# Attention mask from 12 rows of hash bits, moved by DMA, in place of 64 counted one-hot rows; values ahead of hash and fold

## The reference, cut to what matters

```python
# q, k, v: [2, 8, 768, 64]; proj: [64, 6]
q_bits = (q @ proj > 0); k_bits = (k @ proj > 0)
mask = q_bucket[:, :, :, None] == k_bucket[:, :, None, :]   # bucket: the 6 bits as a number
scores = where(mask, scale * q @ k.T, -1e9)
scores = scores - max(scores, axis=-1)
attn = exp(scores); attn = attn / (sum(attn) + 1e-9)
x = attn @ v
...
# x as [1536, 512]: the best of 8 experts by x @ w_gate + bias[modality], relu(x @ w1) @ w2,
# scaled by the gate; then softplus(x @ w_in) @ w_out
```

## Time and profile before

| what | us |
|---|---|
| median of 3 runs (788.20 to 788.98) | 788.89 |
| the profiled execution's own time | 788.01 |
| its span on the core | 786.2 |
| TensorE busy | 738.3 |
| VectorE busy | 580.2 |
| ScalarE busy | 516.8 |
| GpSimd busy | 322.9 |

### The profile page before, as it was taken

The page is one execution under the profiler, slowest core; times in us unless marked ns, Lnnn a source line. Parts: engine busy times, 40 slices in busy tenths (PEclk is TensorE's granted clock), DMA queues, the critical chain, the costliest instruction groups (busy, mean ns, idle before and its releaser), DMA issues.

```text
span 786.2 us, 13234 instructions
## 1 busy us (share of the span) xinstructions
PE 738.3 (94%) x4030; PEld 621.3 (79%) x4030; DVE 580.2 (74%) x841; ACT 516.8 (66%) x938; POOL 322.9 (41%) x281
## 2 busy tenths in 40 slices
PE   5999999999999668999999999999999999999995
PEld 4888888888889556887878887878888788878884
DVE  4999898998999646714989135278888788887884
ACT  5888888888888534635888245365656666566562
POOL 8666546664662270000000000045545664557544
PEclk9999999999999969999999999999999999999999
DMA  6453101220000251503989000023323523234221
GB/s 214 180 172 114 50 30 40 82 89 30 30 10 1 90 142 40 214 0 120 333 315 355 0 0 28 0 61 101 107 83 103 157 85 107 82 105 146 95 81 53
DMA packets 36142, 79.52 MB, mean 101 GB/s; under 512 B 4112, under 2 KB 7056, under 8 KB 36112
## 3 DMA queue, kind: packets, MB, share of 16 engines
q1 hardware_dynamic: 33328, 71.71, 27.0%
q0 software_dynamic: 1920, 6.69, 2.6%
q10 hardware_dynamic: 864, 0.76, 0.3%
HBM read 72.46 MB, written 6.68 MB: 101 GB/s over the span
## 4 chain that ended last, share of the span: by engine, by line
PE 75%; DVE 9%; ACT 7%; issue 5%; POOL 1%; DMA 1%; ACTq 1%; DVEq 0%; POOLq 0%
PE psA L1373 16%; PE psA L1300 11%; PE ps L1173 6%; PE psA L1387 6%; PE psA L1389 5%; PE psA L1388 5%; PE psA L1160 5%; PE psA L1148 5%; PE ps L1182 3%; DVE w1l L968 3%; PE ps L1320 2%; PE ps L1321 2%; PE ps L1324 2%; PE psA L1309 2%; ACT w1h L626 2%
## 5 line engine op out<-in xcount | busy, mean ns | idle before, releaser
L502 POOL TENSOR_TENSOR hres<-hexp,hres 128x512 f32<-128x512 f32 x48 | 62.2, 1296 | 323.3 <-DVE hres L1049 323.2
L821 DVE TENSOR_TENSOR pTl<-psA,pTh 128x384 fp32r<-128x384 f32 x192 | 98.0, 551 | 18.7 <-ACT pTh L573 17.7
L573 ACT ACTIVATE pTh<-psA 128x384 fp32r<-128x384 f32 x192 | 83.9, 490 | 37.5 <-PE psA L1160 36.8
L1148 PE MATMUL psA<-K,Q 128*128 128x384 f32 x384 | 92.6, 364 | 2.0 <-POOLq L408 2.0
L814 DVE TENSOR_REDUCE negmax<-psA 128x1 f32<-128x768 f32 x96 | 91.1, 948 | 2.8 <-PE psA L1148 2.8
L564 ACT ACTIVATE probs<-psA,negmax 128x768 f32<-128x768 f32 x96 | 87.0, 907 | 4.9 <-DVE negmax L814 4.1
L987 DVE SCALAR_TENSOR_TENSOR hTl<-psA,hTh 128x512 fp32r<-128x512 f32 x34 | 23.5, 692 | 90.2 <-ACT hTh L661 90.2
L738 ACT ACTIVATE habs<-psA 128x512 f32<-128x512 f32 x48 | 28.7, 598 | 81.5 <-PE psA L1373 81.4
L1160 PE MATMUL psA<-ident,probs 128*128 128x128 f32 x576 | 80.1, 275 | 0.7 <-DVE pTl L821 0.6
L1003 DVE TENSOR_TENSOR wil<-rawi,wih 128x512 fp32r<-128x512 f32 x48 | 80.2, 1673 | 0.0
L1387 PE MATMUL psA<-woh,sh 128*128 128x512 f32 x192 | 75.4, 392 | 2.4 <-DVE sl L1057 2.3
(11 more groups left out here) (165 smaller groups left out, 1665.7 us busy)
## 6 DMA issues: line engine op xcount, KB each, us to landing
w2s<-in_moe_w SPq DMA_DIRECT2D x8, 2048.0 KB, 8.9
w1s<-in_moe_w SPq DMA_DIRECT2D x8, 2048.0 KB, 9.0
rawi<-in_moe_w_in SPq DMA_DIRECT2D x48, 256.0 KB, 2.7
rawo<-in_moe_w_out SPq DMA_DIRECT2D x48, 256.0 KB, 2.8
raw<-in_qk SPq DMA_DIRECT2D x16, 384.0 KB, 3.1
vs<-in_v SPq DMA_DIRECT2D x16, 192.0 KB, 2.4
x_rows<-X SPq DMA_DIRECT2D x1, 1728.0 KB, 6.0
x_rows<-X SPq DMA_DIRECT2D x1, 1512.0 KB, 5.9
```

What stands on the lines that cost most here:

```text
L573: nc.scalar.activation(pTh[u // TPGR % 2][:, g * TPH:(g + 1) * TPH, u % TPGR * P:(u % TPGR + 1) * P], psA[2][:, g, 0:HALF].rearrange("p (t ...
L821: V.tensor_tensor(pTl[u // TPGR % 2][:, g * TPH:(g + 1) * TPH, cols], psA[2][:, g, 0:HALF].rearrange("p (t n) -> p t n", t=TPH), pTh[u // ...
L1148: last = T.matmul(psA[u % 2][:, h, 0:HALF], qs[par][:, cols], ks[par][:, h * HALF:(h + 1) * HALF], start=start, stop=not start)
```

## The change

Twelve rows take the place of the 64. The projection now has 24 columns: for a query the six projections and the six negated ones, for a key the negated and then the plain ones. `take_bits` compares with a bound for each partition and multiplies by a worth for each partition: 2^100 for query rows, 1 for key rows. The products of a query's 12 rows with a key's 12 rows add up to 2^100 times the number of bits that differ. So q is scaled by -1/8 instead of 1/8, scores are negated, a penalty is added instead of a bonus, and the row pass limits every score to 2^100, writes it back to PSUM, and keeps the row's minimum; exp runs with scale -1.

The bits leave VectorE as fp32 in four strips; SyncE moves them with eight transfers of 12 x 192 values for each head (`move_rows`) into partitions 64 to 75 of Q2 and K2, whose other rows are zeroed once at the start. `one_q`, `one_k`, `count_codes` and the table are gone. On TensorE the values now come before hash and fold. At the start both hashes run before the first scores, four memsets (64 x 768) and a small sign flip of the projection precede them on VectorE, and the first K2 subtraction moves from GpSimd to VectorE. The core of the diff (left out: buffer places, the host's table, sign of the scale on GpSimd, the lines that bring inputs):

```diff
@@ -42,6 +42,8 @@
 PENALTY = 2.0 ** 100
+ROWS = 2 * NBITS
+MOVED = 16 * 2 * PIECES
 TPGR = 3
@@ -302,10 +303,24 @@
+            def move_rows(i, par):
+                sp.wait_ge(bits_ready, i + 1)
+                if i >= 2:
+                    sp.wait_ge(scores_done, i * TPB - TPB)
+                for x, rows in enumerate((Q2, K2)):
+                    for n in range(PIECES):
+                        at = n * STRIP + x * ROWS
+                        sp.dma_start(rows[par][D:D + ROWS, n * SHARE:(n + 1) * SHARE].bitcast(F32), bits[par][at:at + ROWS, :]
+                                     ).then_inc(rows_in[par], 16)
             load_raw(0, 0)
...
             load_v(1, 1)
+            sp.wait_ge(zeroed, 4)
+            move_rows(0, 0)
+            move_rows(1, 1)
@@ -319,6 +334,8 @@
             for i in range(2, HEADS):
+                if i >= 4:
+                    move_rows(i - 2, i % 2)
                 load_raw(i, i % 2)
@@ -327,6 +344,8 @@
+            for i in range(HEADS - 2, HEADS):
+                move_rows(i, i % 2)
             sp.wait_ge(x_ready, PAIRS - 2)
@@ -547,22 +561,13 @@
-            def one_k(i, par, h):
-                act.wait_ge(count_done, i * 2 + h + 1)
-                if not (type(i) is int and i < 2):
-                    act.wait_ge(scores_done, i * TPB - TPB)
-                src = psA[2][D:P, h, 0:HALF] if type(i) is int and i == 0 else ps7[D:P, 0:HALF]
-                nc.scalar.activation(K2[par][D:P, h * HALF:(h + 1) * HALF], src, ACT.Sign,
-                                     bias=negpops[D:P, :]).then_inc(onek_ready, 1)
             def exponents(s, u):
...
                 nc.scalar.activation(probs[u % 2][:, :].rearrange("p (a n) -> p a n", a=2), psA[u % 2][:, :, 0:HALF],
-                                     ACT.Exp, bias=negmax[:, u % 4:u % 4 + 1],
+                                     ACT.Exp, bias=negmax[:, u % 4:u % 4 + 1], scale=-1.0,
                                      accum_out=sums[:, u % SUMS:u % SUMS + 1]).then_inc(exp_done, 1)
@@ -601,14 +602,10 @@
             high_k(0, 0)
-            nc.scalar.activation(Q1[0][0:D, :], raw[0][0:D, :], ACT.Copy, scale=SCALE).then_inc(first_high, 1)
-            act.wait_ge(codes_in, 16)
-            for h in range(2):
-                one_k(0, 0, h)
+            nc.scalar.activation(Q1[0][0:D, :], raw[0][0:D, :], ACT.Copy, scale=-SCALE).then_inc(first_high, 1)
+            high_k(1, 1)
             exponents(0, 0)
-            high_k(1, 1)
             exponents(1, 1)
-            one_k(1, 1, 0)
             body(0, first=True)
@@ -796,23 +793,14 @@
                 if not (type(i) is int and i < 2):
-                    dve.wait_ge(count_done, i * 2 - 2)
-                V.tensor_scalar(bits[par][:, :], ps7[:, 0:SHARE], 0.0, None, ALU.is_gt).then_inc(bits_ready, 1)
-            def one_q(i, par, h):
-                dve.wait_ge(count_done, i * 2 + h + 1)
-                if not (type(i) is int and i < 2):
-                    dve.wait_ge(scores_done, i * TPB - TPB)
-                src = psA[2][0:D, h, 0:HALF] if type(i) is int and i == 0 else ps7[0:D, 0:HALF]
-                V.tensor_scalar(Q2[par][D:P, h * HALF:(h + 1) * HALF], src, pops[0:D, :], PENALTY,
-                                ALU.is_equal, ALU.mult).then_inc(oneq_ready, 1)
+                    dve.wait_ge(rows_in[par], i // 2 * MOVED if type(i) is int else (i - par) * (MOVED // 2))
+                V.tensor_scalar(bits[par][:, :], ps7[:, 0:SHARE], bound, worth, ALU.is_ge, ALU.mult).then_inc(bits_ready, 1)
...
                 dve.wait_ge(scores_done, s + 1)
-                V.tensor_reduce(negmax[:, u % 4:u % 4 + 1], psA[u % 2][:, :, 0:HALF], AX.XY, ALU.max,
-                                negate=True).then_inc(max_done, 1)
+                V.tensor_scalar(psA[u % 2][:, :, 0:HALF], psA[u % 2][:, :, 0:HALF], PENALTY, PENALTY, ALU.min, ALU.min,
+                                accum_out=negmax[:, u % 4:u % 4 + 1]).then_inc(max_done, 1)
@@ -877,19 +860,22 @@
+            for x in (Q2, K2):
+                for par in range(2):
+                    V.memset(x[par][D:P, :].bitcast(F32), 0.0).then_inc(zeroed, 1)
+            dve.wait_ge(proj_in, 16)
+            V.tensor_scalar(proj2[:, NBITS:3 * NBITS], proj2[:, NBITS:3 * NBITS], -1.0, None, ALU.mult).then_inc(proj_ready, 1)
             dve.wait_ge(raw_in[0], 16)
-            V.tensor_scalar(qs[0][0:D, :], raw[0][0:D, :], SCALE, None, ALU.mult).then_inc(first_scaled, 1)
-            dve.wait_ge(codes_in, 16)
+            V.tensor_scalar(qs[0][0:D, :], raw[0][0:D, :], -SCALE, None, ALU.mult).then_inc(first_scaled, 1)
             take_bits(0, 0)
+            dve.wait_ge(k_high, 1)
+            V.tensor_tensor(K2[0][0:D, :], raw[0][D:P, :], K1[0][D:P, :].bitcast(F32), ALU.subtract).then_inc(k_split, 1)
             dve.wait_ge(first_scaled, 1)
...
             V.tensor_tensor(Q1[0][D:P, :], qs[0][0:D, :], Q1[0][0:D, :].bitcast(F32), ALU.subtract).then_inc(first_low, 1)
-            for h in range(2):
-                one_q(0, 0, h)
+            take_bits(1, 1)
             row_max(0, 0)
-            take_bits(1, 1)
             row_max(1, 1)
-            one_q(1, 1, 0)
             body(0, 0, first=True)
@@ -1104,42 +1090,24 @@
                 pe.wait_ge(raw_in[par], (i // 2 + 1) * 16 if type(i) is int else (i - par) * 8 + 16)
-                if type(i) is int and i == 1:
-                    pe.wait_ge(bits_ready, 1)
-                elif type(i) is int and i == 2:
-                    pe.wait_ge(oneq_ready, 4)
-                    pe.wait_ge(onek_ready, 4)
-                elif not (type(i) is int and i == 0):
+                if not (type(i) is int and i == 0):
+                    pe.wait_ge(bits_ready, i)
+                if not (type(i) is int and i < 3):
                     pe.wait_ge(x_ready, i * 2 - 5)
                 for n in range(PIECES):
-                    last = T.matmul(ps7[n * STRIP:(n + 1) * STRIP, 0:SHARE], proj2[:, :], raw[par][:, n * SHARE:(n + 1) * SHARE],
+                    last = T.matmul(ps7[n * STRIP:(n + 1) * STRIP, 0:SHARE], proj2, raw[par][:, n * SHARE:(n + 1) * SHARE],
                                     start=True, stop=True)
                 last.then_inc(z_done, 1)
-            def count_codes(i, par, h):
-                pe.wait_ge(bits_ready, i + 1)
-                if type(i) is int and i == 0:
-                    dst = psA[2][:, h, 0:HALF]
-                else:
-                    dst = ps7[:, 0:HALF]
-                    if h == 1:
-                        pe.wait_ge(oneq_ready, i * 2 + 1)
-                        pe.wait_ge(onek_ready, i * 2 + 1)
-                    elif not (type(i) is int and i < 3):
-                        pe.wait_ge(x_ready, i * 2 - 4)
-                for n in range(2):
-                    last = T.matmul(dst[:, n * SHARE:(n + 1) * SHARE], codes_of[h * 2 + n], bits[par][:, :], start=True, stop=True)
-                last.then_inc(count_done, 1)
...
                     pe.wait_ge(q_split, i * 3 + 3)
+                    if type(i) is int and i == 0:
+                        pe.wait_ge(first_low, 1)
                     pe.wait_ge(k_split, i + 1)
-                    pe.wait_ge(oneq_ready, i * 2 + 2)
-                    pe.wait_ge(onek_ready, i * 2 + 2)
+                    pe.wait_ge(rows_in[par], (i // 2 + 1) * MOVED if type(i) is int else (i - par) * (MOVED // 2) + MOVED)
                 if not (type(s) is int and s < 2):
@@ -1178,6 +1146,8 @@
                 pe.wait_ge(oT_ready, G + 1)
+                if not (type(G) is int and G == 0):
+                    pe.wait_ge(x_ready, G)
                 for t in range(TPGR):
@@ -1188,41 +1158,23 @@
                     par = (u // TPB + 1) % 2
-                    ahead = not (last and u >= TPB)
                     if not (last and u >= 2 * TPB - 2):
                         scores(s + 2, (u + 2) % (2 * TPB), i if u % TPB < TPB - 2 else i + 1)
-                    if u % TPB == 0 and ahead:
-                        count_codes(i + 1, par, 1)
-                    if u % TPB == 1 and not (first and u < 7):
-                        if ahead:
-                            pe.wait_ge(oneq_ready, i * 2 + 4)
-                            pe.wait_ge(onek_ready, i * 2 + 4)
-                        else:
-                            pe.wait_ge(x_ready, j * 4 + (u - 7) // TPGR)
+                    if not (first and u < 4):
+                        values(j * 4 + (u - 4) // TPGR, (u - 4) // TPGR % 4, (u - 4) % TPGR)
+                    if u % TPGR == 1 and not (first and u < 7):
+                        if u % TPB == 4 and not last:
+                            pe.wait_ge(bits_ready, i + 3)
                         fold_out(j * 4 + (u - 7) // TPGR, (u - 7) // TPGR % 4, j * 2 + (u - 7) // TPB)
...
                         hash_qk(i + 2, 1 - par)
-                    if u % TPB == 4 and not (first and u < 7):
-                        if not last:
-                            pe.wait_ge(bits_ready, i + 3)
```

(63 more changed lines are left out.)

12 lines of the change are left out of this document (1 added, 11 removed).

## The result

The changed kernel takes 774.33 us (median of 4 runs, 774.06 to 774.78) against 788.62 for the kernel before beside it: a ratio of 0.982, 95% interval 0.9803 to 0.9837. That is 14.3 us less; the forecast was 771.5, in a range of 763.3 to 783.0.

What follows compares the result with a forecast made beforehand. TensorE was taken as the bound, held by waits for writes to `ps7`. 25.6 - 4.9 (ScalarE) - 2.8 (VectorE) - 0.5 (start) = 17.4 us gained, so a median of 771.5 us, range 763.3 to 783.

Steps and rivals of the forecast that it cites:

- the start: First scores at 11.0, 2.1 us later; first transposes 0.1 late, up to 1; 0.5 us taken as loss.
- Counts and waits: TensorE in attention: counts and the waits of hash, counts and fold go, 25.6 us gained at most.
- The last head's tiles: Last head, without mask work: 2.72 us a fold tile, 2.05 a plain one, 13.64 us for six tiles.
- The order as cover for X: TensorE at u % 6 = 1: work moved before hash, 2.05 us, covers its 0.25 us wait for X.
- ScalarE 0.35 and VectorE 0.2 a head: Attention: high_k ahead of ScalarE's copies costs 4.9 us over 14 heads, VectorE being just full 2.8.
- the accumulator: VectorE's row pass: reading out the minimum adds up to 0.207 us a pass, 1.24 us a head.
- Moving the rows: SyncE: eight transfers issued at 0.33 us each, 2.6 us, landing 2.4 after the last; cost nothing.
- The slower one: Rival at the row pass: PSUM write takes its own slot, 0.79 us a pass; about 834 us; chance 0.06.
- Late rows: Rival on the row transfers: each starts only when the one ahead landed, 21.6 us a head; 868 us; chance 0.02.
- VectorE takes over: Rival on VectorE: accumulator read puts 1.24 us a head on the path; 786 us, half of it 778; chance 0.13.
- All is hidden: Rival in attention: accumulator costs nothing and high_k is covered; 763.3 to 767 us; chance 0.11.

Runs made afterwards that it cites:

- the two edits: Changed kernel with high_k at u % 6 = 4 instead of 5 and the 128x3 sum written to PSUM: 768.11 us, ratio 0.9753.
- The two-queue start: Changed kernel with the key rows of heads 0 and 1 issued by ScalarE's queue while SyncE issues the query rows: 771.25 us, ratio 0.9775.

## Why the prediction was right, and where it was off

The direction and the range held. The forecast of 17.4 us against 14.3 measured is off mainly in one term of the sum, the start; two other parts came out near their number although their reasons were wrong.

*Counts and waits (25.6 us): right for fold and counts, wrong for hash.* The idle times before fold and counts are gone, and a head is 14.75 us in place of 15.99, where 14.7 was worked out. The last head's tiles gave the floor that the others then came close to. But the 25.6 hold 3.6 us for hash waiting on X, and of these 14 pauses of 0.25, 3.5 us, stayed. From scores to scores the tile with hash took 2.71 us before and takes 2.66 after (138.95 to 141.61). That the head still came near 14.7 is in part luck: the two tiles with a count took 5.04 us before (168.71 to 173.75), 0.94 more than two plain ones, where the sum took 0.79 for them.

*The order as cover for X: needed, but not for the reason told.* The prediction set the wait of 0.25 against the cover, and that 0.25 was the pause. With the old order and without passes and counts hash waits 0.6 us, and the order brings 5.6 us. That before it hardly waited for X because the counts' and the fold's waits held TensorE elsewhere in the head is likely, but no run shows it.

*ScalarE 0.35 and VectorE 0.2 a head: the sum right by luck, the structure wrong.* Together 0.55 was taken; the two edits bring a head from 14.75 to 14.21, 0.54. But the two were added as if they stood one after the other. They are nearly parallel: with either edit alone a head is 14.65, so each chain by itself costs 0.44, and both together 0.54. And VectorE's cause was not the accumulator, priced at 0.207 us a pass and 1.24 a head: the step behind the pass starts no later for it (0.87 us against 0.86 in the run with a plain reduction). It was the 128x3 sum, whose row grew from a median of 0.160 us to 0.613. Before, it met GpSimd's cast or scaling in some places only (up to 0.686); now it does in most. The prediction didn't look at that row at all.

*Moving the rows: no cost in the steady heads, as told, by a thinner margin.* The step that failed is the price of an issue: 0.33 us, from a load of 128 partitions. It measured 0.71 to 0.78, so eight take 6.1 us. In a steady head SyncE had that room: the next qk load goes out 6.76 us behind the v load, as before, with 0.3 us left. Where a weight load stands ahead it goes out 0.3 late (7.08 behind the v load at 56.53), and in the head at 145.18, where an `x_rows` transfer does, 10.4 behind it; that head still takes 14.65 us.

*The start (0.5 us): wrong, and it is the miss.* The first scores were predicted at 11.0, with 0.33 an issue, and started at 13.93. The bits themselves came at 6.36, 0.4 later than the 5.95 taken, since hash waited for the sign flip and started at 4.94 instead of 4.08. From the first issue at 6.45, eight of 0.78 end at 12.7, and the scores start 1.3 behind that. So the issues took 3.6 us more than the 2.6 of the sum, the bits 0.4 more, and the landing, taken as 2.4, 1.1 less, which hid a part of the error. First transposes 3.35 late instead of 0.5 is 2.85 us. By the profiled spans (13.8 us shorter, 17.4 forecast) 3.6 are missing: these 2.85, 0.6 in the heads (17.3 where 25.6 - 4.9 - 2.8 = 17.9 was taken), and about 0.2 behind the last fold, which no run explains. The two-queue start won 2.0 back by its profile, 3.1 by the medians.

*Rivals.* The slower one, a PSUM write with a slot of its own, needed about 1.75 us a pass; it was 0.956. Late rows: only at the start, where the scores waited for the last transfer. VectorE takes over: not by the accumulator. All is hidden: no, but the run with `high_k` early and `den` in PSUM comes near it.

## What to carry to other kernels

Price a transfer's issue by its own form: the first use of a value that comes by eight transfers from one queue waits for eight issues, and where the start hangs on it, a second queue shortens that (here from 6.2 us to 3.4). When one edit moves an idle time instead of removing it, look for a second chain of the same length at the same place and try both edits together before giving either up. Before an idle time is put down to a wait, see whether it is also there where that wait cannot be. A step of three values can last until another engine's instruction ends; look at the spread of short rows, not at their mean alone.

## What the runs showed of the hardware

A pass that limits 768 fp32 values from PSUM back into PSUM with a minimum in its accumulator took 0.956 us, 8 ns more than a plain reduction, with a read-out of 0.142 that didn't lengthen the kernel.

VectorE's 128x3 scalar step from SBUF to SBUF took 0.16 us at its shortest and up to 0.70 beside GpSimd in the kernel after. Two places there (VectorE, then GpSimd):

```profile
131.20 0.70 DVE L818 TENSOR_SCALAR den<-sums 128x3 f32<-128x3 f32 x1
...
138.84 0.45 DVE L818 TENSOR_SCALAR den<-sums 128x3 f32<-128x3 f32 x1
```

```profile
131.04 0.83 POOL L431 CAST Q<-qs 64x768 fp32r<-64x768 f32 x1
...
137.13 2.12 POOL L412 TENSOR_SCALAR qs<-raw 64x768 f32<-64x768 f32 x1
```

The two rows end at 131.90 and 139.29, GpSimd's at 131.87 and 139.25. With its output in PSUM the same step took 0.204. The Trainium skill ("SBUF — State Buffer", section "Who interferes with whom") says that a scalar step in a two-port mode takes a port pair shared with GpSimd, and that whoever issues first blocks the other for a whole instruction; this trace agrees.

An issue on SyncE's queue took 0.33 us for a q and k or v load of 128 partitions from HBM, 0.71 to 0.78 for 12 partitions from SBUF to SBUF, and 0.59 to 0.62 for 16.

The 128x32 weight loads of hash had 0.25 us of idle time ahead of them in all 14 heads of the kernel after, and 0.30 to 0.31 behind them, whether the profile names X for it or nothing.
